# Half 0's channel mix: the right half of w_k by three split products instead of plain fp32 ones

## The reference

```
    x_prev = np.concatenate([np.zeros((B, 1, D)), x[:, :-1, :]], axis=1)
    xk = mu_k * x + (1.0 - mu_k) * x_prev
    xr = mu_r * x + (1.0 - mu_r) * x_prev
    k = np.maximum(xk @ w_k, 0.0)
    v = k * k @ w_v
    r = 1.0 / (1.0 + np.exp(-(xr @ w_r)))
    return (r * v)
```

## Time and profile before

| | |
|---|---|
| median of 3 runs | 531.36 us (530.97 to 531.49) |
| the profiled execution | 531.16 us, of which its span 529.3 us |
| PE busy | 517.5 us, 98% of the span |
| PEld (weight loads) busy | 480.2 us, 91% |
| DVE busy | 325.3 us, 61% |
| ACT busy | 287.8 us, 54% |
| POOL busy | 119.3 us, 23% |
| mean granted TensorE clock | 0.997 of full speed |

### The profile page before, as it was taken

One profiled execution on the slowest core, in us unless ns is written; L12 is line 12 of the kernel. 1 busy time (PEld: TensorE's weight loads), 2 busy tenths in 40 slices (PEclk: granted clock), 3 DMA queues, 4 the chain that ended last, 5 costly groups with the idle time before them and its releaser, 6 DMA issues.

```text
span 529.3 us, 15349 instructions
## 1 busy us (share of the span) xinstructions
PE 517.5 (98%) x6200; PEld 480.2 (91%) x6203; DVE 325.3 (61%) x815; ACT 287.8 (54%) x783; POOL 119.3 (23%) x145
## 2 busy tenths in 40 slices
PE   7799999999999999999989999999999999999997
PEld 6477999999999999999989999988998899889985
DVE  5769985658658566657644745883397039807910
ACT  4389288296394592690970724761474048416720
POOL 9229972022031040140221682000000000000000
PEclk9999999999999999999998999999999999999999
DMA  9983423343243341332106126001300130010011
GB/s 203 191 276 56 72 76 63 65 94 65 62 90 65 94 70 41 82 63 45 48 2 249 46 80 213 4 0 61 109 1 12 68 109 0 19 61 0 0 40 59
DMA packets 98622, 39.07 MB, mean 74 GB/s; under 512 B 90952, under 2 KB 91134, under 8 KB 98558
## 3 DMA queue, kind: packets, MB, share of 16 engines
q1 hardware_dynamic: 93992, 33.09, 25.3%
q0 software_dynamic: 1824, 4.44, 2.6%
q10 hardware_dynamic: 2742, 0.66, 0.8%
HBM read 28.72 MB, written 9.44 MB: 72 GB/s over the span
## 4 chain that ended last, share of the span: by engine, by line
PE 85%; DVE 5%; ACT 3%; POOL 3%; issue 2%; DMA 1%; POOLq 0%; DVEq 0%; ACTq 0%
PE ps L769 19%; PE ps L779 19%; PE ps L663 8%; PE ps L664 8%; PE ps L665 8%; PE ps L714 6%; PE ps L715 6%; PE ps L716 6%; PE ps L608 2%; PE ps L550 2%; POOL vs L356 2%; ACT sm L817 2%; DMA vs<-in_v_dram 1%; PE ps L592 1%; DVE diff L1065 1%
## 5 line engine op out<-in xcount | busy, mean ns | idle before, releaser
L486 POOL TENSOR_TENSOR k_lo<-k,k_hi 128x288 fp32r<-128x288 f32 x64 | 60.9, 956 | 192.2 <-ACT k_hi L836 192.2
L1243 DVE SCALAR_TENSOR_TENSOR cbuf<-hbuf,cols_c,cbuf 128x576 f32<-128x576 f32 x64 | 52.4, 819 | 63.5 <-ACT cbuf L939 62.4
L714 PE MATMUL ps<-k_hi,wb_hi 128*128 128x288 f32 x256 | 76.8, 300 | 0.0
L715 PE MATMUL ps<-k_lo,wb_hi 128*128 128x288 f32 x256 | 76.2, 298 | 0.0
L716 PE MATMUL ps<-k_hi,wb_lo 128*128 128x288 f32 x256 | 76.1, 297 | 0.0
L663 PE MATMUL ps<-xk_hi,wa_hi 128*128 128x288 f32 x224 | 67.0, 299 | 0.0
L664 PE MATMUL ps<-xk_lo,wa_hi 128*128 128x288 f32 x224 | 66.1, 295 | 0.0
L665 PE MATMUL ps<-xk_hi,wa_lo 128*128 128x288 f32 x224 | 66.1, 295 | 0.0
L779 PE MATMUL ps<-wb_hi,g_hi 128*128 128x512 f32 x144 | 57.5, 399 | 0.0
L779 PE MATMUL ps<-wb_hi,g_lo 128*128 128x512 f32 x144 | 56.8, 394 | 0.0
L779 PE MATMUL ps<-wb_lo,g_hi 128*128 128x512 f32 x144 | 56.5, 392 | 0.0
(11 more groups left out here) (107 smaller groups left out, 1166.5 us busy)
## 6 DMA issues: line engine op xcount, KB each, us to landing
x2d<-x2s SPq DMA_DIRECT2D x8, 576.0 KB, 3.1
x2raw<-x2d SPq DMA_DIRECT2D x4, 1152.0 KB, 5.5
out_dram<-ob SPq DMA_DIRECT2D x16, 256.0 KB, 2.0
raw<-in_q_dram SPq DMA_DIRECT2D x96, 36.0 KB, 2.0
raw<-in_k_dram SPq DMA_DIRECT2D x96, 36.0 KB, 1.9
wk_raw<-in_moe_w_k_dram SPq DMA_DIRECT2D x4, 512.0 KB, 9.2
wv_raw<-in_moe_w_v_dram SPq DMA_DIRECT2D x4, 512.0 KB, 5.1
ws<-in_moe_w_in_dram POOLq DMA_DIRECT2D x4, 512.0 KB, 7.3
```

Of the source, the lines that this page charges most:

```text
L486: nc.gpsimd.tensor_tensor(k2_lo[:, m], k2[:, m % K2RING], k2_hi[:, m].bitcast(F32), ALU.subtract).then_inc(k2_done, 1)
L714: nc.tensor.matmul(dst, wb_hi[:, f, cols], k2_hi[:, f, :], start=(f == 0), stop=False)
L715: nc.tensor.matmul(dst, wb_hi[:, f, cols], k2_lo[:, f, :], start=False, stop=False)
L1243: nc.vector.scalar_tensor_tensor(out=c, in0=h[:, o:o + S], scalar=conv[:, o, m:m + 1], in1=c, op0=ALU.mult, op1=ALU.add).then_inc(conv_ste ...
```

## The change

Tiles 4 to 7 of w_k (columns 512 to 1023, the right half, from `PLAIN` on) are done in half 0 as split products. For that

- ScalarE copies the right half of each of the four row tiles of `wk_raw` to `wa_hi` early (`high_right`), two between the exponentials of half 0 and the copy of the strided output, two behind that copy, and then copies half 0's `xk_raw` to `xk_hi` in four pieces; `high_w1` later copies only the left half;
- GpSimd subtracts the right halves as four instructions ahead of its first `low_k2`, once all four pieces of `xk_raw` are mixed; `low_w1` later does only the left half;
- VectorE takes `xk_lo` of half 0 in four pieces between `lay_k(1, False)` and `mask_and_max(1, 0)`;
- `xk_raw` moves out of the place of `xk_hi` to that of `raw`, so half 2's first load into `raw` also waits for the fourth w_k tile and for `xk_lo`;
- the zero matmuls ahead of the attention change from 23 of 224 columns to 9 of 512, and a later group from 8 to 6.

```diff
-    WARM_START, WARM_COLS, WARM_SLOT = 23, 224, 4
+    WARM_START, WARM_COLS, WARM_SLOT = 9, 512, 4
...
+        PLAIN_M = FT // 2
+        PLAIN = P * PLAIN_M
...
+            if h == 2 and not strided:
+
+                wait(eng, tile_done, PLAIN_M)
+                wait(eng, xk_done, KT)
...
                 if i < WK_IN:
+
+                    cols = PLAIN
                     pool.wait_ge(w1_hi_act, WV_POOL + i + 1)
-                    pool.wait_ge(tile_done, FT)
+                    pool.wait_ge(tile_done, PLAIN_M)
...
+            pool.wait_ge(k_mixed, KT)
+            for i in range(WK_IN):
+                _, raw_w, hi, lo = weights1[i]
+                pool.wait_ge(wk_right_hi, i + 1)
+                nc.gpsimd.tensor_tensor(lo[:, :, PLAIN:], raw_w[:, :, PLAIN:], hi[:, :, PLAIN:].bitcast(F32),
+                                        ALU.subtract).then_inc(wk_right_lo, 1)
...
-                if h == 0 and s < FT:
+                if h == 0 and s < PLAIN_M:
                     plain_w_k(s, range(EARLY_T if s < EARLY_M else 0, KT)).then_inc(tile_done, 1)
...
+                    if h == 0 and s == PLAIN_M:
+                        pe.wait_ge(wk_right_lo, KT)
...
-                            xk_done if s == 0 else None, KT * h,
+                            xk_done if s == (0 if h else PLAIN_M) else None, KT * h,
...
-            keep_warm(2 * WARM_SLOT)
+            keep_warm(WARM_SLOT + WARM_SLOT // 2)
...
+            def high_right(i):
+                _, raw_w, hi, _ = weights1[i]
+                act.wait_ge(w1_loaded[i], 16)
+                nc.scalar.copy(hi[:, :, PLAIN:], raw_w[:, :, PLAIN:]).then_inc(wk_right_hi, 1)
...
             exps(0, 2)
+            high_right(0)
+            high_right(1)
...
                 copied.then_inc(first_copied, 1)
+            high_right(2)
+            high_right(3)
+            for t in range(KT):
+                act.wait_ge(k_mixed, t + 1)
+                nc.scalar.copy(xk_hi[:, t], xk_raw[:, t]).then_inc(xk_hi_done, 1)
...
                     if h == 0 and slot == TURN[0]:
                         lay_k(1, False)
+                        for t in range(KT):
+                            low_xk(0, t)
```

More of the change, by code:

```diff
@@ L132, in attention_channel_mix_gated_conv @@
         diff = sb("diff", [P, KT, HALF], stack=mix)
+        xk_hi = sb("xk_hi", [P, KT, HALF], F32R, mix)
         with ExitStack() as early:
-            xk_raw = sb("xk_raw", [P, KT, HALF], stack=early)
             xr_raw = sb("xr_raw", [P, KT, HALF], stack=early)
-        xk_hi, xr_hi, xk_lo, xr_lo = (
-            sb(n, [P, KT, HALF], F32R, mix) for n in ("xk_hi", "xr_hi", "xk_lo", "xr_lo"))
+        xr_hi, xk_lo, xr_lo = (sb(n, [P, KT, HALF], F32R, mix) for n in ("xr_hi", "xk_lo", "xr_lo"))
         rt = sb("rt", [P, 2, HALF], stack=mix)
@@ L150, in attention_channel_mix_gated_conv @@
         with ExitStack() as att:
+            with ExitStack() as early:
+                xk_raw = sb("xk_raw", [P, KT, HALF], stack=early)
             raw = sb("raw", [P, 2, 2 * PAIRS, JH, STRIDE], stack=att)
@@ L191, in attention_channel_mix_gated_conv @@
         wv_hi_dve, wv_lo_dve = sem("wv_hi_dve"), sem("wv_lo_dve")
+        wk_right_hi, wk_right_lo = sem("wk_right_hi"), sem("wk_right_lo")
         raw_loaded = [sem(f"raw_loaded_{n}") for n in ("local", "strided")]
@@ L465, in low_w1 @@
                 _, raw_w, hi, lo = weights1[i]
+                cols = hi.shape[2]
                 if i < WK_IN:
+                    cols = PLAIN
                     pool.wait_ge(w1_hi_act, WV_POOL + i + 1)
-                    pool.wait_ge(tile_done, FT)
+                    pool.wait_ge(tile_done, PLAIN_M)
                 elif i < WR_IN:
@@ L475, in low_w1 @@
                 n = LOW_COLS
-                pieces = [(x, y) for x in range(hi.shape[1]) for y in range(0, hi.shape[2], n)]
+                pieces = [(x, y) for x in range(hi.shape[1]) for y in range(0, cols, n)]
                 for x, y in pieces:
@@ L676, in mlp @@
                     bank = ps[:, t % 4, 0:HALF]
-                if h == 0 and s < FT:
+                if h == 0 and s < PLAIN_M:
                     plain_w_k(s, range(EARLY_T if s < EARLY_M else 0, KT)).then_inc(tile_done, 1)
-                elif h == 0 and s < FT + KT:
+                elif h == 0 and FT <= s < FT + KT:
                     n = s - FT
@@ L858, in high_w1 @@
                 act.wait_ge(w1_loaded[i], 16)
-                nc.scalar.copy(hi, raw_w).then_inc(w1_hi_act, 1)
+                cols = slice(0, PLAIN if i < WK_IN else DM)
+                nc.scalar.copy(hi[:, :, cols], raw_w[:, :, cols]).then_inc(w1_hi_act, 1)
+            def high_right(i):
+                _, raw_w, hi, _ = weights1[i]
+                act.wait_ge(w1_loaded[i], 16)
+                nc.scalar.copy(hi[:, :, PLAIN:], raw_w[:, :, PLAIN:]).then_inc(wk_right_hi, 1)
             act.sem_inc(h_done, FT)
             act.sem_inc(g_hi_done, FT)
-            act.sem_inc(xk_hi_done, KT)
             act.sem_inc(xr_hi_done, KT)
@@ L1074, in low_xk @@
                 wait(dve, xk_hi_done, KT * h + t + 1)
-                if t == 0:
+                if h and t == 0:
                     wait(dve, tile_done, TILES * (h - 1) + FT)
-                nc.vector.tensor_tensor(xk_lo[:, t], mixed[:, t], xk_hi[:, t].bitcast(F32),
+                nc.vector.tensor_tensor(xk_lo[:, t], mixed[:, t] if h else xk_raw[:, t], xk_hi[:, t].bitcast(F32),
                                         ALU.subtract).then_inc(xk_done, 1)
@@ L1083, in mix_r @@
                 wait(dve, diffed, KT * h + t + 1)
-                wait(dve, xk_done, KT * h + t + 1)
+                if h:
+                    wait(dve, xk_done, KT * h + t + 1)
                 into = mixed[:, t] if h else xr_raw[:, t]
```

1 line of the change is left out of this document (removed).

## The result

| | before | after |
|---|---|---|
| median, us | 531.36 (529.57 to 533.22, 20 runs) | 533.9 (532.3 to 539.58, 20 runs) |
| profiled span, us | 529.3 | 532.1 |
| ratio | 1 | 1.0055 [1.0041, 1.0069] |

The kernel is slower by 0.55%, 2.5 us, and outside the forecast range (529.7 to 532.7). What was priced at 0.15 of chance, a stall that takes TensorE's clock along, is what happened.

What follows compares the result with a forecast made beforehand. The path over VectorE's mixing and ScalarE's `relu` into slot 8 of half 1 decides: 1.2 us late less 0.95 back, +0.25 on 531.16 gives 531.4, stated as 531.6 us because the profiled run lies 0.2 under the median; range 529.7 to 532.7.

Steps and rivals of the forecast that it cites:

- VectorE: where it turns: Half 0, ahead of block (1, local)'s maxima: four `xk_lo` cost 3.2 us, maxima come 2.05 us later.
- The second term that failed: TensorE behind the 2.0 us stall in slot 3's k transposes: the sum added no loss for the clock.
- the second rival: Slot 3's 2.0 us stall takes TensorE's clock down, costing 1.7 us: 533.1 us; chance 0.15.
- old wait: TensorE's wait for ScalarE's rectified tile at slot 8 of half 1: 0.6 us to spare.
- the prediction's two paths: Into slot 8 of half 1: TensorE's comes out at 0, the one over VectorE and ScalarE +0.25 us and decides.
- TensorE's saving: Slots 4 to 7 of half 0: four split tiles at 1.61 us instead of 1.97, 1.4 us less.
- ScalarE: Half 0's casts and `xk_hi` pieces end at 27.0 us, before the q copy at 27.16: cost 0, 0.15 to spare.
- GpSimd: Four subtractions of 512 columns from 26.0 us: 5.8 to 9.4 us, taken as 6.8; low wait only in dearest case.
- The zero matmuls and the loads: Zero matmuls lie under the transfer of the values, half 2's load waits far later than slot 4: both cost 0.
- The mixing pair of half 1: VectorE's pair moves from 66.24 to 67.44 us, just free of GpSimd: 0.94 instead of 1.90 us.
- The first rival: VectorE is hardly slowed, `xk_lo` of half 0 costs 1.6 us: faster, 530.4 us; chance 0.26.
- The third: TensorE's old clock fall around 275 us disappears, giving back 1.7 us: faster, 529.9 us; chance 0.13.

Runs made afterwards that it cites:

- experiment 4: Changed kernel, but GpSimd's four subtractions wait until `xk_lo` is complete instead of until `xk_raw` is mixed; 532.85 us, ratio 1.0024.
- experiment 6: Changed kernel plus 24 matmuls on zeros on TensorE ahead of the wait for the maxima; 529.78 us, ratio 0.9973.
- experiment 5: Changed kernel with GpSimd's right halves in two instructions of 2 x 512 columns; 534.98 us, ratio 1.0074, four runs.
- experiment 7: Changed kernel, GpSimd in 256-column pieces, three beside the mixing, five after `xk_lo`; two `xk_lo` pieces ahead of the k copy; 530.75 us, ratio 0.9996.
- experiment 3: Changed kernel with the old zero matmuls again (23 of 224 columns, later group of 8); 532.45 us, ratio 1.0036.
- experiment 8: 32 zero matmuls of 32 columns added near 18 us: to the kernel before 531.12 us, the changed kernel 531.03, the version keeping GpSimd and VectorE apart 526.84.
- experiments 2: Changed kernel with the four `xk_lo` pieces behind the maxima of block (1, local) instead of ahead; 531.98 us, ratio 1.0022.
- before + 32: Kernel before the change plus 32 zero matmuls of 32 columns on TensorE ahead of half 0's first w_k products; 531.12 us, ratio 0.9994.

## Why the prediction was wrong

**The step that failed** is the price of `xk_lo` in "VectorE: where it turns". It was 4 x 0.80 us, from a row in which GpSimd works in pieces of 256 columns; the new ones have 512. The price follows the length of GpSimd's pieces once they are varied:

| GpSimd beside it | four `xk_lo` |
|---|---|
| idle | 1.55 us |
| 128 columns | 2.44 |
| 256 | 3.25 |
| 512 | 4.65 |

In the changed kernel the single pieces took 0.79, 1.52, 1.52 and 1.04 us and ended at 29.5, 30.9, 32.4 and 33.3 us, each about 0.35 us after GpSimd had gone from one instruction to the next (29.12, 30.58, 32.02, 32.99). So VectorE gets one such instruction in for each GpSimd instruction, and pays GpSimd's length, here 1.45 us. With 256 columns the two engines also keep step (0.85 us from one GpSimd instruction to the next, 0.81 us for a piece of `xk_lo`); with 128 columns not quite (0.53 and 0.61 us). That is how the numbers read; no run shows the mechanism inside the chip. My row was right for its pieces, and the price did not carry over to pieces twice as long.

The Trainium skill, GPSIMD Engine Reference, section 8, says that GpSimd contends with VectorE instructions that have two SBUF inputs, and with those in a 2-port perf mode. The traces agree for two inputs (pairs 0.94 to 3.05 us, the copies of the local k from PSUM 0.81 or 0.82 in all). They add that an instruction with one SBUF input can be hit as well: `nb<-mx` took 1.30 us in experiment 4 and 0.72 with 256 columns, against 0.17. Whether it ran in such a mode no run shows.

**What followed from it.** A stall of 3.2 us instead of 2.0 (maxima at 33.26, not 31.85). The second term that failed is the clock, which the sum held at full speed; with 2.0 us I had taken its fall for unlikely. Of the 2.83 us by which the segment grew, the fall is one half (1.42 us, experiment 6) and the longer delay the other (1.41 us). Without the fall the time would have been near 532.8 us, an estimate from 531.4 and 1.4; so the price alone brings the time to the edge of the range (532.7), and the clock carries it past.

In the traces a wait for the maxima of 0.9 and 1.7 us left the clock alone, those of 3.2 us took it down in three traces, and so did the wait of 2.2 us in experiment 4; the wait of 2.8 us in experiment 5 did not. The idle times of 1.6 to 2.1 us near 277 us took it down in eight traces of nine (not in experiment 7, 1.93 us). So the length of an idle time alone does not decide, and whether a stall of 2.0 us in slot 3 would have taken the clock along is open. On its own row, an idle time of 1.9 us with a fall behind it, the second rival deserved more than 0.15. Its price was 533.1 us; the clock cost 1.4 us where it took 1.7 from the earlier trace rows, and the delay itself is larger, hence 533.9. The Trainium skill, TensorE: Matmul & The Clock Gate, section "HAM oscillation", describes waits between bursts of matmuls behind which the clock is back at half, and the trace agrees with that (granted clock 0.51 behind the stall). The waits of its example are longer than the forecast one, so it does not bear out what the prediction drew from it, that this case is likelier.

**The sum as it came out, at slot 8 of half 1.** TensorE: +3.2 stall, +1.4 clock, -1.4 cheaper tiles, -0.6 old wait, +0.2 from the start of `xr_raw`, together 2.8 against a measured 3.0. ScalarE's `relu` is 2.75 us later (81.93 to 84.68), so both paths arrive within 0.3 us of each other (`relu` ends at 85.08, the slot starts at 85.38), as the prediction's two paths had it, but nearly 3 us later. On the second path the exponentials of the block are 2.65 us late (34.88 against 32.23), not 1.2, and the mixing pair 3.74 (69.98 against 66.24); the cheaper pair gives 1.0 back.

**Right:** 
- *TensorE's saving.* Twelve split matmuls in a tile, 0.13 us apart where the clock is full, no plain tile left in slots 4 to 7.
- *ScalarE.* The eight new casts (0.56 and 0.36 us each) end at 27.0 us, and the q copy behind them starts at 27.32 having waited 0.34 for TensorE: no cost.
- *GpSimd.* 5.81 us, within 5.8 to 9.4 though not at my 6.8. No wait on `wa_lo` in slot 4.
- *The zero matmuls and the loads:* nothing in the trace (experiment 3; TensorE waits nowhere for half 2's q and k).
- *The mixing pair of half 1* is free of GpSimd: 0.90 us at 69.98, with GpSimd done at 69.4. ScalarE works without a pause from there to the `relu`, so without this 1.0 us the `relu` would have ended near 86.1 us, by estimate 0.7 us behind TensorE.

The first rival (`xk_lo` cheap) had the better idea of the size: with `xk_lo` out of the way the segment is 0.7 us shorter (experiment 7). The third (the old fall gone) did not happen by itself; experiment 8 shows it could be had, and that it was worth twice what I gave it (3.5 to 4.0 us against 1.7), since the gap goes along with the fall.

## What to carry to other kernels

Price an instruction that runs beside GpSimd by the length of GpSimd's instructions, not by how busy it is: shorter pieces cost GpSimd 1 to 2.6 us here and gave VectorE 1.4 to 2.2 us back where it was on the path. Before an instruction is put into a free-looking place of an engine, look whose wait comes right behind it; here a subtraction needed in slot 4 stood ahead of maxima needed in slot 3. And compare traces by segments with a common anchor: idle times of TensorE that no semaphore explains moved the whole by up to 4 us and hid or faked the effect of an edit. Where a row says "issue", compare its end with the ends of the other engines' work that the instruction needs: in experiments 2 and 4 a copy and a subtraction ended 0.1 us ahead.

## What the runs showed of the hardware

- TensorE can idle in the middle of a block of matmuls that waits for nobody (the row says "issue"), at a place fixed by its list: between 275 and 281 us in all nine versions without added matmuls or with 16 more (1.6 to 2.1 us); with 24 zero matmuls more it was 0.5 us, with 32, or 16 and the old group, there was none. With the clock's fall behind it that cost 3.5 to 4.0 us.
- What it waits for is not recorded, but a refill of the instruction stream fits. In all ten traces with the idle time TensorE goes on 2.4 to 2.7 us after a transfer of 16 KB on the DMA queue that the page lists as "q8 instruction" has started (before: 274.67 and 277.32 us; changed: 277.40 and 279.77). The two early gaps of before + 32 end 2.6 and 2.4 us behind such a start as well (14.31 and 20.97 us).
- GpSimd's subtraction of 128x512 in fp32 takes 1.45 us from one to the next beside `xk_lo`, and 1.3 us in experiment 4, where it meets other work. GpSimd loses some 12% by that comparison, while the `xk_lo` beside it takes three times as long.
- A fall of the clock comes and goes between runs of one kernel, and each is a step of about 1.6 us in its time: the kernel before stood at 1.000 in 11 of 35 runs and under 0.9955 in 4. A trace shows one of these cases.
